# Turning the attention probabilities as two halves of 64 queries on the upper and lower rows of the array

## The chip, the cores and the metric

The kernel runs on one core of a Trainium2 chip. The metric is the device time of one execution, in microseconds. Times come from repeated runs; the profile is one further execution recorded by the hardware profiler.

## The reference

Pooled attention over 8 batches, 8 heads, 576 queries and head size 64, with keys and values averaged over groups of 8 (72 keys), then two layers of 4608 tokens, 512 wide, with a hidden width of 2048:

```python
k_p = k.reshape(B, H, Sp, pool, D).mean(axis=3)      # Sp = 72
v_p = v.reshape(B, H, Sp, pool, D).mean(axis=3)
scores = scale * np.matmul(q, k_p.transpose(0, 1, 3, 2))
attn = exp(scores - max); attn = attn / (sum(attn) + 1e-09)
x = (attn @ v_p) as 4608 x 512
h = x @ w_in;  g = h * (1.0 / (1.0 + np.exp(-h)));        x = g @ w_out
h = x @ w_in2; g = h * np.clip(h + 3.0, 0.0, 6.0) / 6.0;  out = g @ w_out2
```

## The kernel before, in words

The two layers are worked in four passes (two halves of the hidden width per layer) of nine steps each, `STEPS` = 36. A step takes one block of 512 tokens: first eight chunks (the product with `w_in`, by a fast scheme with seven block products instead of eight, in two fp32r parts each; lines 628 to 630), then 32 units (the product with `w_out`, three matmuls each; lines 714 to 716 in layer one, 720 to 722 in layer two).

The attention of batch s+1 is laid between the chunks and units of step s, for s = 0 to 6. A table written out by hand (`PLAN`, and `PLAN_FIRST` for step 0) says at which place of a step which event stands. A batch is five query tiles, `ROWS = [128, 128, 128, 128, 64]`: four full ones and a fifth of 64 queries. The events of a tile are "qt" (queries transposed, line 729), "s" (scores, line 736), "exp", "norm" (VectorE, lines 1332 to 1338), "pt" (`transpose_p`, line 745) and "pv" (`values`, line 753). The attention of batch 0 stands ahead of all steps, in `attend_first` (`first_turn` calls `transpose_p`), and the fifth tile of batch 0 is finished inside step 0.

`transpose_p` turns the probabilities `p_sb` of a tile, 8 heads of (queries x 72 keys), so that the keys lie on partitions. Each head is one fp32 transpose on TensorE: the probabilities are the weights (queries x 72 columns), the identity is the moving operand. Heads 0 to 3 go to one PSUM bank, heads 4 to 7 to a second one, and `pt_done` counts up when a bank is full:

```python
for g in range(2):
    for h in range(GH):
        last = nc.tensor.transpose(banks[g][:SP, h * P:h * P + rows], p_sb[:rows, tile % CT, GH * g + h, :],
                                   ident[:rows, :rows])
    last.then_inc(pt_done, 1)
```

ScalarE copies each bank to `pt` (line 1044; line 1094 for batch 0), and `values` then multiplies each head by the pooled values, even heads into the lower and odd heads into the upper 64 partitions of one bank, which are the two column halves of the array. ScalarE then copies that result to `x_raw` (line 1061) where the next step needs it, and to `x_out` (line 1066), which it sends to DRAM itself (line 1068).

In `PLAN` the first full tile is turned at place U+9 and its values follow at U+12; the other full tiles and the fifth are turned right behind the values of the tile before (U+12, U+15, U+18, U+21), and their own values follow three units later. In `PLAN_FIRST` the distance between "pt" and "pv" is two units from tile 0 on.

Of the kernel before, what the change touches and what calls it, by code (L numbers as in the profile page):

```python
# [10 lines left out]
B, H, S, D = 8, 8, 576, 64  # L11
POOL = 8
SP = S // POOL
DM = H * D
DF = 2048
P = 128
# [2 lines left out]
HB = BLK // 2  # L19
NB = B * S // BLK  # L20
GH = H // 2

# [8 lines left out]
CT = 5  # L33
# [140 lines left out]
def build(nc, q, k, v, w_in1, w_out1, w_in2, w_out2, out):  # L174
# [15 lines left out]
    with ctx:  # L190
        def sb(stack, name, shape, dt=fp32):
            return stack.enter_context(nc.sbuf_tensor(name, shape, dt))
# [26 lines left out]
        pt_first = sb(first_q, "pt_first", [SP, 2, H, P])  # L219
# [15 lines left out]
        ident = sb(att, "ident", [P, P])  # L235
# [5 lines left out]
        p_sb = sb(att, "p_sb", [P, CT, H, SP])  # L241
        pt = sb(att, "pt", [SP, H, P])
# [17 lines left out]
        banks = ab + zw + xy + acc  # L260
        first_q_bank = [ab[0], xy[0], xy[1], acc[0], acc[1]]
        first_s_banks = [(ab[0], ab[1]), (xy[0], zw[0]), (xy[1], zw[1]), (ab[0], ab[1]), (acc[0], acc[1])]
        first_p_banks = [(xy[0], zw[0]), (xy[1], zw[1]), (xy[0], zw[0]), (xy[1], zw[1])]
# [35 lines left out]
        pt_done = sem("pt_done")  # L299
# [69 lines left out]
        def first_value(h, heads=1):  # L369

            at = h % GH * D
            return w1_sum0[:SP, 2 + h // GH, 3, at:at + heads * D]

# [248 lines left out]
        def _(pe):  # L622
# [116 lines left out]
                        last.then_inc(s_done, 1)  # L739

            def transpose_p(tile, banks):
                rows = ROWS[tile % CT]
                for g in range(2):
                    for h in range(GH):
                        last = nc.tensor.transpose(banks[g][:SP, h * P:h * P + rows], p_sb[:rows, tile % CT, GH * g + h, :],
                                                   ident[:rows, :rows])
                    last.then_inc(pt_done, 1)

# [151 lines left out]
        def _(act):  # L900
# [117 lines left out]
            def attend(e):  # L1018
                kind, t = e[0], e[1]
                if kind == "kt":  # L1020
                    act.wait_ge(kt_done, t + 1)
                    if t == 1:
                        act.wait_ge(s_done, 2 * CT)
                    src = ab[0][:, :NK * SP].rearrange("p (j r) -> p j r", r=SP)
                    nc.scalar.copy(kt[:D, :, :SP], src[:D])
                    nc.scalar.copy(kt[D:, :, SP:], src[D:]).then_inc(bank_read[0], 1)
                elif kind == "qt":
                    rows = ROWS[t % CT]
                    n = t - CT
                    bank = banks_of(e)[0]  # L1030
                    act.wait_ge(qt_done, t + 1)
                    if t + 2 < TILES:
                        act.dma_start(q_raw[:ROWS[(t + 2) % CT], n % 2], q_rows(t + 2)).then_inc(q_loaded[n % 2], 16)
                    nc.scalar.copy(qt[:, :, :rows], banks[bank][:].rearrange("p (j r) -> p j r", r=P)[:, :, :rows])\
                        .then_inc(bank_read[bank], 1)
                elif kind == "exp":
                    exps(t, e[2])
                elif kind == "pt":
                    rows = ROWS[t % CT]
                    for g in range(2):  # L1040
                        bank = acc[g] if t == FIRST else banks[banks_of(e)[g]]
                        copied = first_pt_copied if t == FIRST else bank_read[banks_of(e)[g]]
                        act.wait_ge(pt_done, 2 * t + g + 1)
                        nc.scalar.copy(pt[:, GH * g:GH * (g + 1), :rows],
                                       bank[:SP].rearrange("r (h p) -> r h p", p=P)[:, :, :rows]).then_inc(copied, 1)
                elif kind == "pv":
                    b, c = t // CT, t % CT
                    rows = ROWS[c]
                    if t == FIRST:
                        bank, copied, count = acc[0], first_x_copied, CT  # L1050
                    else:
                        n = banks_of(e)[0]
                        bank, copied, count = banks[n], bank_read[n], BEFORE["pv", t, n] + 1
                    src = bank[:].rearrange("p (j r) -> p j r", r=P)
                    act.wait_ge(pv_done, t + 1)
                    if DIRECT[t]:
                        at, first, width = DIRECT[t]
                        act.wait_ge(x_split, 4 * max(b, 1))
                        if b <= 1:
                            act.wait_ge(x_first_stored, 64)  # L1060
                        nc.scalar.copy(x_raw[:, :, at:at + width], src[:, :, first:first + width]).then_inc(x_direct, 1)
                    if t > FIRST:
                        act.wait_ge(x_stored, 16 * (t - FIRST))
                    else:
                        act.wait_ge(x_first_stored, 64)
                    nc.scalar.copy(x_out[:, :, :rows], src[:, :, :rows]).then_inc(copied, 1)
                    act.wait_ge(copied, count)
                    act.dma_start(x_rows[:, :, b * S + c * P:b * S + c * P + rows], x_out[:, :, :rows])\
                        .then_inc(x_stored, 16)

            def attend_first():
                act.wait_ge(ident_ready, 2)
                act.wait_ge(zeroed, 1)
                nc.scalar.activation(ssum[:, 0, :1], ident[:, :1], ACT.Exp)

                def copy_q(c):
                    rows = ROWS[c]
                    act.wait_ge(qt_done, c + 1)
                    nc.scalar.copy(qt_fifth[:, :, :rows] if c == FIRST else qt_first[:, c],
                                   first_q_bank[c][:].rearrange("p (j r) -> p j r", r=P)[:, :, :rows])\  # L1080
                        .then_inc(first_qt_copied, 1)

                def exp(c):
                    rows = ROWS[c]
                    act.wait_ge(first_s_read, 2 * c + 2)
                    nc.scalar.activation(p_sb[:rows, c % CT], p_sb[:rows, c % CT], ACT.Exp, scale=float(D) ** -0.5 / POOL)\
                        .then_inc(exp_done, 1)

                def copy_p(c):
                    for g in range(2):  # L1090
                        act.wait_ge(pt_done, 2 * c + g + 1)
                        if c >= 2:
                            act.wait_ge(pv_done, c - 1)
                        nc.scalar.copy(pt_first[:, c % 2, GH * g:GH * (g + 1), :],
                                       first_p_banks[c][g][:SP].rearrange("r (h p) -> r h p", p=P))\
                            .then_inc(first_pt_copied, 1)

                def copy_x(c):
                    act.wait_ge(pv_done, c + 1)
                    src = first_v_bank[c][:].rearrange("p (j r) -> p j r", r=P)  # L1100
                    nc.scalar.copy(x_raw[:, :, c * P:(c + 1) * P], src).then_inc(first_x_copied, 1)
                    if c >= 2:
                        nc.scalar.copy(x_out[:, 2 * (c - 2):2 * (c - 1), :], src[:, 0:2]).then_inc(first_x_kept, 1)

                copy_q(0)
                act.wait_ge(kt_done, 1)
                src = acc[1][:, :NK * SP].rearrange("p (j r) -> p j r", r=SP)
                nc.scalar.copy(kt[:D, :, :SP], src[:D]).then_inc(first_kt_copied, 1)
                nc.scalar.copy(kt[D:, :, SP:], src[D:]).then_inc(first_kt_copied, 1)
                copy_q(1)  # L1110
                copy_q(2)
                exp(0)
                copy_q(3)
                exp(1)
                exp(2)
                copy_p(0)
                act.wait_ge(v_summed, 2)
                nc.scalar.copy(first_value(GH, GH), acc[1][:SP, 2 * P:]).then_inc(v_copied, 1)
                copy_p(1)
                round_w1(0, 0)  # L1120
                exp(3)
                copy_x(0)
                round_w1(0, 1)
                copy_p(2)
                copy_x(1)
                copy_p(3)
                round_x_first()
                copy_x(2)
                copy_q(FIRST)
                copy_x(3)  # L1130
                round_x_second()
                act.wait_ge(k_next_summed, 2)
                act.wait_ge(kt_done, 1)
                nc.scalar.copy(k_pool[:, GH:], ab[0][:SP, 2 * P:].rearrange("r (h d) -> r h d", d=D)).then_inc(k_next_copied, 1)
                round_x_last()
                round_w1(0, 2)

            attend_first()
            for s in range(STEPS):
                ps, blk = divmod(s, NB)  # L1140
                for place in range(END + 1):
# [7 lines left out]
                    else:  # L1149
# [4 lines left out]
                        if place in (2, 3, 6, 7):  # L1154
                            p = CHUNKS[place][1]
# [274 lines left out]
```

## Time and profile before

| | us |
|---|---|
| median of 3 runs (1703.26 to 1704.2) | 1703.68 |
| the profiled execution's own time | 1705.6 |
| its span, first to last instruction | 1703.8 |
| PE busy | 1686.2 (99%) |
| weight loads busy | 1519.0 (89%) |
| VectorE busy | 1040.7 (61%) |
| ScalarE busy | 726.5 (43%) |
| GpSimd busy | 351.9 (21%) |

An engine's busy time counts overlapping instructions once. A matmul's recorded duration is the time through the pipeline, so what a group of matmuls costs is read from the distance of starts in the timeline: from the start of the group to the start of what follows. In shapes such as "64*72 64x64" the weights are 64 partitions by 72 columns, and the moving operand is 64 partitions by 64 columns. An fp32 matmul that isn't a transpose is recorded twice, once for each pair of its passes, so the eight heads of `values` stand as x16.

### The profile page before, as it was taken

Reading aid. Unit: us, or ns where it says so; the run is one execution under the profiler, and the core shown is the slowest. Engines: PE = TensorE matmul, PEld = TensorE weight load, DVE = VectorE, ACT = ScalarE, POOL = GpSimd, SP = SyncE. Lnnn points to the kernel's source line nnn. Section 1 sums busy time; section 2 is a strip of 40 time slices with the busy share of each in tenths; the row PEclk is TensorE's granted clock in tenths of the full one; section 3 lists DMA queues with packets and bytes.
Section 4 is the critical chain, followed back from the end, with each engine's and each line's share of the span. In section 5 each row is a group of like instructions: output and inputs, shape, how many; then the busy total and the mean of one; then the engine's idle time right before and its main releaser. Section 6 shows DMA issues by size and latency. Waiting matters only on the chain.

```text
span 1703.8 us, 27465 instructions
## 1 busy us (share of the span) xinstructions
PE 1686.2 (99%) x11096; PEld 1519.0 (89%) x11096; DVE 1040.7 (61%) x1568; ACT 726.5 (43%) x1183; POOL 351.9 (21%) x443
## 2 busy tenths in 40 slices
PE   8999999999999999999999999999999999999999
PEld 7888988998899999999999899999998899999998
DVE  7757656656656555555557655555557666666664
ACT  4655555555544533333334434343335433333332
POOL 6655534634206300000006200000006200000000
PEclk7899999999999999999999999999999999999999
DMA  8243333443212322222223211111112322222221
GB/s 211 77 119 102 109 97 106 113 120 101 76 47 99 124 75 75 75 75 75 77 79 130 91 53 54 53 53 54 44 61 88 117 77 79 77 78 78 78 79 49
DMA packets 129838, 145.83 MB, mean 86 GB/s; under 512 B 47536, under 2 KB 74416, under 8 KB 129712
## 3 DMA queue, kind: packets, MB, share of 16 engines
q1 hardware_dynamic: 79968, 127.95, 22.9%
q10 hardware_dynamic: 49744, 16.13, 3.8%
q8 instruction: 88, 1.44, 0.4%
q14 instruction: 38, 0.31, 0.1%
HBM read 96.86 MB, written 47.19 MB: 85 GB/s over the span
## 4 chain that ended last, share of the span: by engine, by line
PE 95%; DVE 3%; ACT 1%; issue 1%; DMA 0%; POOL 0%; ACTq 0%; DVEq 0%; POOLq 0%
PE zw L628 8%; PE zw L629 8%; PE zw L630 8%; PE xy L628 6%; PE xy L630 6%; PE xy L629 6%; PE acc L714 6%; PE acc L716 5%; PE acc L715 5%; PE acc L720 4%; PE acc L721 4%; PE acc L722 4%; PE att L720 4%; PE att L722 4%; PE att L721 4%; PE att L716 2%
## 5 line engine op out<-in xcount | busy, mean ns | idle before, releaser
L1217 DVE TENSOR_TENSOR g_lo<-g_raw,g_hi 128x1024 fp32r<-128x1024 f32 x144 | 194.8, 1355 | 9.4 <-ACT g_raw L920 9.4
L908 ACT COPY x_sum<-xy 128x256 f32<-128x256 f32 x144 | 52.4, 365 | 293.8 <-PE xy L630 293.5
L1182 DVE TENSOR_TENSOR x_sum<-xy,x_sum 128x256 f32<-128x256 f32 x144 | 60.5, 420 | 189.6 <-ACT x_sum L908 189.6
L628 PE MATMUL xy<-xr_hi,w1r_hi 128*128 128x256 f32 x576 | 166.0, 288 | 0.6 <-DVE x_sum L1182 0.6
L533 POOL TENSOR_TENSOR w_sum<-w_raw 128x256 f32<-128x256 f32 x16 | 16.6, 1036 | 715.9 <-DMA w_raw<-in_moe_w_in_dram 715.9
L630 PE MATMUL xy<-xr_hi,w1r_lo 128*128 128x256 f32 x576 | 163.4, 284 | 0.0
L629 PE MATMUL xy<-xr_lo,w1r_hi 128*128 128x256 f32 x576 | 163.3, 283 | 0.0
L714 PE MATMUL acc<-g_hi,w_hi 128*128 128x512 f32 x400 | 162.2, 405 | 0.0
L1206 DVE TENSOR_TENSOR g_raw<-zw,x_sum 128x512 f32<-128x512 f32 x144 | 99.0, 688 | 95.6 <-PE zw L630 95.6
L716 PE MATMUL acc<-g_hi,w_lo 128*128 128x512 f32 x400 | 156.4, 391 | 0.0
L715 PE MATMUL acc<-g_lo,w_hi 128*128 128x512 f32 x400 | 156.2, 390 | 0.0
L547 POOL TENSOR_TENSOR kv_stage<-kv_stage 72x256 f32<-72x256 f32 x104 | 86.6, 833 | 159.7 <-DMA kv_stage<-in_v_dram 131.6
L1232 DVE SCALAR_TENSOR_TENSOR g_raw<-relu,g_raw 128x768 f32<-128x768 f32 x72 | 70.8, 983 | 72.9 <-ACT relu L937 72.9
L720 PE MATMUL acc<-w_hi,g_hi 128*128 128x512 f32 x288 | 113.0, 392 | 0.0
L628 PEld LDWEIGHTS xy<-xr_hi,w1r_hi 128*128 128x128 f32 x576 | 110.7, 192 | 2.4 <-DVE x_sum L1182 1.0
L721 PE MATMUL acc<-w_lo,g_hi 128*128 128x512 f32 x288 | 112.8, 392 | 0.0
L722 PE MATMUL acc<-w_hi,g_lo 128*128 128x512 f32 x288 | 112.5, 391 | 0.0
L720 PE MATMUL att<-w_hi,g_hi 128*128 128x512 f32 x288 | 112.0, 389 | 0.0
L721 PE MATMUL att<-w_lo,g_hi 128*128 128x512 f32 x288 | 112.0, 389 | 0.0
L722 PE MATMUL att<-w_hi,g_lo 128*128 128x512 f32 x288 | 112.0, 389 | 0.0
L629 PEld LDWEIGHTS xy<-xr_lo,w1r_hi 128*128 128x128 f32 x576 | 110.7, 192 | 1.4
L630 PEld LDWEIGHTS xy<-xr_hi,w1r_lo 128*128 128x128 f32 x576 | 110.7, 192 | 0.0
(209 smaller groups left out, 4882.1 us busy)
## 6 DMA issues: line engine op xcount, KB each, us to landing
partial<-y_stage SPq DMA_DIRECT2D x72, 256.0 KB, 2.1
y_part<-partial SPq DMA_DIRECT2D x18, 1024.0 KB, 5.9
x_raw<-first_layer_t SPq DMA_DIRECT2D x18, 1024.0 KB, 7.8
x_raw<-attended_t SPq DMA_DIRECT2D x10, 1024.0 KB, 8.2
first_layer_t<-y_stage SPq DMA_DIRECT2D x36, 256.0 KB, 2.0
out_dram<-y_stage SPq DMA_DIRECT2D x36, 256.0 KB, 2.0
w_raw<-in_moe_w_in_dram SPq DMA_DIRECT2D x16, 512.0 KB, 4.2
kv_stage<-in_v_dram SPq DMA_DIRECT2D x56, 144.0 KB
```

The costliest lines, as they stand in the source:

```text
L547: nc.gpsimd.tensor_tensor(src[:, :4 * D], src[:, :4 * D], src[:, 4 * D:], ALU.add).then_inc(kv_added, 1)
L628: nc.tensor.matmul(dst, s_hi[i], m_hi[i], start=first and i == 0, stop=False, skip_group_check=True)
L629: nc.tensor.matmul(dst, s_hi[i], m_lo[i], start=False, stop=False, skip_group_check=True)
L630: last = nc.tensor.matmul(dst, s_lo[i], m_hi[i], start=False, stop=i == 1, skip_group_check=True)
L714: nc.tensor.matmul(dst, w[0], g[0], start=f == 0, stop=False)
L715: nc.tensor.matmul(dst, w[0], g[1], start=False, stop=False)
L716: last = nc.tensor.matmul(dst, w[1], g[0], start=False, stop=f == NF - 1)
L720: nc.tensor.matmul(dst, g[0], w[0], start=f == 0, stop=False)
L721: nc.tensor.matmul(dst, g[0], w[1], start=False, stop=False)
L722: last = nc.tensor.matmul(dst, g[1], w[0], start=False, stop=f == NF - 1)
L1206: nc.vector.tensor_tensor(dst, src, u2[:, p % 2].unsqueeze(1).to_broadcast([P, 2, HB]), ALU.add)\
L1217: nc.vector.tensor_tensor(g_lo[:, p], g_raw[:, p % 2], g_hi[:, p].bitcast(fp32), ALU.subtract)\
```

## The change

A full tile is turned head by head as two transposes: queries 0 to 63 (partitions 0 to 63 of `p_sb`) into bank 0, queries 64 to 127 (partitions 64 to 127) into bank 1. Each bank then holds all eight heads, 64 columns a head. `pt_done` counts up twice at the end of the tile instead of once in the middle and once at the end. ScalarE's two copies of a tile read 72 x 512 contiguous columns as before and write eight runs of 64 with a step of 128. The fifth tile of 64 queries is turned as before, with its heads packed 64 columns apart in the bank.

```diff
+HP = P // 2
...
             def transpose_p(tile, banks):
                 rows = ROWS[tile % CT]
+                if rows == P:
+                    for h in range(H):
+                        for g in range(2):
+                            half = slice(g * HP, (g + 1) * HP)
+                            last = nc.tensor.transpose(banks[g][:SP, h * HP:(h + 1) * HP], p_sb[half, tile % CT, h, :],
+                                                       ident[half, half])
+                            if h == H - 1:
+                                last.then_inc(pt_done, 1)
+                    return
                 for g in range(2):
                     for h in range(GH):
-                        last = nc.tensor.transpose(banks[g][:SP, h * P:h * P + rows], p_sb[:rows, tile % CT, GH * g + h, :],
+                        last = nc.tensor.transpose(banks[g][:SP, h * HP:(h + 1) * HP], p_sb[:rows, tile % CT, GH * g + h, :],
                                                    ident[:rows, :rows])
                     last.then_inc(pt_done, 1)
...
                         act.wait_ge(pt_done, 2 * t + g + 1)
-                        nc.scalar.copy(pt[:, GH * g:GH * (g + 1), :rows],
-                                       bank[:SP].rearrange("r (h p) -> r h p", p=P)[:, :, :rows]).then_inc(copied, 1)
+                        src = bank[:SP].rearrange("r (h p) -> r h p", p=HP)
+                        if rows == P:
+                            nc.scalar.copy(pt[:, :, HP * g:HP * (g + 1)], src).then_inc(copied, 1)
+                        else:
+                            nc.scalar.copy(pt[:, GH * g:GH * (g + 1), :HP], src[:, :GH]).then_inc(copied, 1)
...
-                        nc.scalar.copy(pt_first[:, c % 2, GH * g:GH * (g + 1), :],
-                                       first_p_banks[c][g][:SP].rearrange("r (h p) -> r h p", p=P))\
+                        nc.scalar.copy(pt_first[:, c % 2, :, HP * g:HP * (g + 1)],
+                                       first_p_banks[c][g][:SP].rearrange("r (h p) -> r h p", p=HP))\
                             .then_inc(first_pt_copied, 1)
```

The turns keep their places on TensorE. Below is TensorE's order in step 1, around the values of the first tile and the turn of the second (`xy` and `zw` are PSUM banks, `v_pool` the pooled values), first of the kernel before:

```order
L716 MATMUL acc<-g_hi,w_lo 128x512
L753 MATMUL xy<-pt,v_pool 64x128 x8
L745 MATMUL zw<-ident,p_sb 72x128 x8
L714 MATMUL acc<-g_hi,w_hi 128x512
L715 MATMUL acc<-g_lo,w_hi 128x512
```

and of the changed kernel, whose lines stand one to twelve further down:

```order
L717 MATMUL acc<-g_hi,w_lo 128x512
L765 MATMUL xy<-pt,v_pool 64x128 x8
L750 MATMUL zw<-ident,p_sb 72x64 x16
L715 MATMUL acc<-g_hi,w_hi 128x512
L716 MATMUL acc<-g_lo,w_hi 128x512
```

Eight transposes of 128 columns have become sixteen of 64; both banks there are `zw` banks, written in turn. TensorE's order ahead of the steps, at the first tile of batch 0, where the two banks are `xy0` and `zw0`, was

```order
L821 MATMUL acc<-v_first,ident 72x128 x8
L745 MATMUL xy<-ident,p_sb 72x128 x4
L745 MATMUL zw<-ident,p_sb 72x128 x4
L821 MATMUL acc<-v_first,ident 72x128 x8
```

and begins in the changed kernel with

```order
L833 MATMUL acc<-v_first,ident 72x128 x8
L750 MATMUL xy<-ident,p_sb 72x64
L750 MATMUL zw<-ident,p_sb 72x64
```

the last two rows eight times over. The other engines keep their order and their waits.

## Rows read from the trace of the kernel before

**Rows 1.** The page: its first part and its chain of waits.
```profile
PE 1686.2 (99%) x11096; PEld 1519.0 (89%) x11096; DVE 1040.7 (61%) x1568; ACT 726.5 (43%) x1183; POOL 351.9 (21%) x443
...
PE 95%; DVE 3%; ACT 1%; issue 1%; DMA 0%; POOL 0%; ACTq 0%; DVEq 0%; POOLq 0%
```

**Rows 2.** Timeline of PE, step 1, second tile: start us, us, engine, line, shapes, count.
```profile
156.21 1.09 PE L753 MATMUL xy<-pt,v_pool 72*64 72x128 f32 x16
157.24 1.07 PE L745 MATMUL zw<-ident,p_sb 128*72 128x128 f32 x8
...
158.37 0.40 PE L715 MATMUL acc<-g_lo,w_hi 128*128 128x512 f32 x1
```

**Rows 3.** The same, step 1, first tile.
```profile
152.95 0.39 PE L716 MATMUL acc<-g_hi,w_lo 128*128 128x512 f32 x1
153.18 1.03 PE L745 MATMUL zw<-ident,p_sb 128*72 128x128 f32 x8
...
154.28 0.39 PE L715 MATMUL acc<-g_lo,w_hi 128*128 128x512 f32 x1
```

**Rows 4.** The same, step 1, fifth tile: its turn behind values.
```profile
168.54 1.09 PE L753 MATMUL xy<-pt,v_pool 72*64 72x128 f32 x16
169.56 0.64 PE L745 MATMUL zw<-ident,p_sb 64*72 64x64 f32 x8
170.13 0.50 PE L714 MATMUL acc<-g_hi,w_hi 128*128 128x512 f32 x1
170.47 0.40 PE L715 MATMUL acc<-g_lo,w_hi 128*128 128x512 f32 x1
```

**Rows 5.** The same, step 1, the fifth tile's values, in two column halves.
```profile
172.07 0.39 PE L716 MATMUL acc<-g_hi,w_lo 128*128 128x512 f32 x1
172.39 0.69 PE L753 MATMUL xy<-pt,v_pool 72*64 72x64 f32 x16
173.01 0.50 PE L714 MATMUL acc<-g_hi,w_hi 128*128 128x512 f32 x1
173.34 0.39 PE L715 MATMUL acc<-g_lo,w_hi 128*128 128x512 f32 x1
```

**Rows 6.** Timeline of PE ahead of the steps: sums of v, undivided array.
```profile
21.08 1.91 PE L821 MATMUL acc<-v_first,ident 72*72 72x128 f32 x16
```

**Rows 7.** Timelines of PE up to 69.8 us and up to 72 us: the same turn.
```profile
69.53 0.47 PE L745 MATMUL acc<-ident,p_sb 64*72 64x64 f32 x5
...
69.53 0.64 PE L745 MATMUL acc<-ident,p_sb 64*72 64x64 f32 x8
```

**Rows 8.** Weight loads by line: ns min/median/max, first and last start, forms.
```profile
L729 PEld LDWEIGHTS xy<-ident,q_raw x32: 134/137/140, 82.0 to 445.3; 64*128 64x128 f32 x28, 128*128 128x128 f32 x4
L745 PEld LDWEIGHTS acc<-ident,p_sb x8: 110/112/113, 69.5 to 69.9; 64*72 64x72 f32 x8
```

**Rows 9.** Timelines of ACT and PE, step 1, second tile, up to its values.
```profile
158.87 1.07 ACT L1044 COPY pt<-zw 72x512 f32<-72x512 f32 x2 [0.45 <-ACT x_out L1066]
...
160.32 0.55 PE L753 MATMUL xy<-pt,v_pool 72*64 72x128 f32 x6
```

**Rows 10.** The same, step 0, third tile.
```profile
102.13 1.07 PE L745 MATMUL zw<-ident,p_sb 128*72 128x128 f32 x8
...
103.76 1.06 ACT L1044 COPY pt<-zw 72x512 f32<-72x512 f32 x2 [0.45 <-ACT x_out L1066]
...
104.97 0.44 PE L753 MATMUL xy<-pt,v_pool 72*64 72x128 f32 x4 [0.37 <-ACT pt L1044]
```

**Rows 11.** Timeline ahead of the steps: PE and DVE, third and fourth tile.
```profile
28.58 1.07 PE L745 MATMUL xy<-ident,p_sb 128*72 128x128 f32 x4 [0.40 <-DVE p_sb L1338]
30.44 1.97 PE L753 MATMUL att<-pt_first,w_sum 72*64 72x128 f32 x16
30.65 1.12 DVE L1338 TENSOR_TENSOR p_sb<-p_sb,ssum 128x576 f32<-128x576 f32 x1
32.34 1.07 PE L745 MATMUL xy<-ident,p_sb 128*72 128x128 f32 x4
36.10 0.69 PE L729 MATMUL acc<-ident,q_fifth 64*128 64x64 f32 x4
36.71 1.97 PE L753 MATMUL att<-pt_first,w_sum 72*64 72x128 f32 x16
```

**Rows 12.** Windows: length, busy time by engine, granted clock, DMA share, GB/s.
```profile
24.40:51.60 27.20, 26.80 (x150) 22.86 (x151) 23.98 (x26) 16.88 (x28) 21.53 (x20) 0.50 0.53 149
65.40:68.60 3.20, 3.20 (x17) 3.20 (x17) 3.20 (x3) 2.65 (x5) 3.12 (x3) 0.50 0.63 158
```

**Rows 13.** Timeline of PE in step 0, where it waits longest.
```profile
64.58 0.66 PE L729 MATMUL att<-ident,q_raw 128*128 128x128 f32 x4 [3.12 <-DVE p_sb L1324]
```

## The prediction

> **What bounds the kernel now.** I read the page first. TensorE is busy 99% of the span, and the chain that ended last is TensorE for 95% of it [rows 1]. So an edit on TensorE counts nearly one for one wherever TensorE doesn't wait, and work on the other engines counts only where TensorE waits for it. The share of busy time says nothing of what a small matmul costs, so next I read TensorE's timeline around each kind of turn, from start to start. In step 1 the second tile's turn starts at 157.24 and the unit that follows has its second matmul at 158.37: 1.13 us for the turn and the first matmul [rows 2]. A first tile, which comes behind a unit and not behind values, takes 1.33 us from the unit's last matmul (152.95) to the next unit's second (154.28) [rows 3]. The fifth tile, 8 transposes of 64 columns on 64 rows, takes 169.56 to 170.47, 0.91 us [rows 4].
>
> There are 32 full tiles: 4 in batch 0, ahead of the steps, and 4 in each of steps 0 to 6.
>
> **What the change does, part by part.**
>
> *The turns of steps 0 to 6.* Eight transposes of 128 columns become sixteen of 64. The number of columns moved is the same, so if the instructions ran one after the other nothing would be won. What can win is that the upper and lower rows work at the same time. No row shows two row halves at work together; the nearest rows show two column halves. Undivided, 16 records of 128 columns take 1.91 us [rows 6]; `values`, 16 such records spread over two column halves, take 1.09 us [rows 2]. So halves of the array do run side by side in this kernel, at almost half the time. `values` of the fifth tile are 16 records of 64 columns in pairs, which is just the shape of the new turn: 0.62 us to the next unit's first matmul, 0.95 us to its second (172.39 to 173.34) [rows 5]. The other end is the fifth tile's turn, which is 8 such transposes in 0.91 us: with a perfect partner for each the new turn costs the same 0.91.
>
> A turn behind values (second to fourth tile) so goes from 1.13 to between 0.91 and 0.95 us: 0.18 to 0.22 saved, I take 0.20. That is little, because the divided array has to be left again: the first matmul behind the fifth tile's turn costs more than behind a full one. Behind the unit's last matmul, the first tile's turn goes from 1.33 us to 1.27 (172.07 to 173.34 is the same passage for `values` [rows 5]), or a little less: 0.06 to 0.10 saved, I take 0.08, since there the array is divided and joined again where before it never was.
>
> The Trainium skill (TensorEngine Tiling (Array Packing), Key Properties) speaks against the change: "Mode switching requires drain". The trace agrees: eight transposes at 0.057 us (below) and a unit's matmul at 0.23 make 0.69 us, and the fifth tile's turn takes 0.91, so passages cost 0.22. Without them 25 turns would save 5.5 us more than the sum below.
>
> *What hides and what doesn't.* `values` of a tile need both of ScalarE's copies. In step 1 the copies of the second tile begin at 158.87, behind the copies of the first tile's result and the sending of it, not behind the turn, and end at 159.94; `values` start at 160.32 [rows 9], 0.38 us later. In step 0 they start at 104.97, and there they wait: the copies end at 104.82, and the shortest distance is 0.15 [rows 10]. So from step 1 on a turn can become shorter by about 0.23 us before TensorE has to wait for ScalarE; the 0.20 just fits. In step 0 the second, third and fourth tile are bound by ScalarE already, and their saving is worth nothing: it comes back as a longer wait for `pt`.
>
> Both counts of `pt_done` now come at the end of the turn. Before, the first bank was full half way; the new turn as a whole ends about when that was, since it needs half the array time, so ScalarE starts no later. Copies have the same 512 columns on 72 partitions: nothing. 256 more instructions and weight loads are in the queue: nothing, since `values` of the fifth tile pass at the same rate.
>
> Sum: 6 steps x 3 tiles x 0.20 = 3.6; 7 first tiles x 0.08 = 0.6; step 0's other three 0. **4.2 us** saved, from 3.7 to 4.7 by the ends.
>
> *The turns of batch 0.* These run at half the clock (0.50 from 24.4 to 51.6) [rows 12]. The first two are followed by waits for VectorE's probabilities and give nothing. The third goes from 28.58 to the values at 30.44: 1.86 us [rows 11]. Four transposes of 64 columns and the passage to `values` take 0.61 there (36.10 to 36.71); with four more pairs at 0.11, twice the full-clock 0.057, the new turn is some 1.05 us. So 0.8 us each for the third and fourth. VectorE's last norm ends at 31.77, while TensorE would be ready at 31.5, so the two are worth 1.4 to 1.6 us of time at half the clock. All up to 51.6 runs at half the clock anyway, so this is 0.7 to 0.8 us of work at full clock. Behind it VectorE and ScalarE are almost fully busy with the first block, and TensorE ends by waiting 3.12 us for VectorE at 64.58 [rows 13]; if nothing passes through them the gain is 0. I take 0.8, ends 0 and 1.6.
>
> Just behind that wait the clock is halved once more for 3.2 us and a little [rows 12], which costs half of that, 1.7 us. If the wait moves, this fall may not come, or another may. That is 1.7 us either way, and not in the sum.
>
> **Sum:** 4.2 + 0.8 = 5.0 us. The profiled execution took 1705.6 us and would become 1700.6; the median of the runs is 1703.7, so 1698.7 us, 0.29% less. A measurement of this kernel tells about 0.2%, 3.4 us, from no change.
>
> **Rivals.**
>
> *The row halves take turns (slower).* If the lower half's transpose can't start while the upper one runs, sixteen transposes pass at the fifth tile's pace. Of one of those turns the first five end after 0.47 us and all eight after 0.64 [rows 7], 0.057 us each, so eight more add 0.45. A turn behind values costs 1.36 instead of 1.13, 0.23 more; a first tile's loses 0.35. 18 x 0.23 + 7 x 0.35 = 6.6, batch 0 about nothing, step 0's others hidden: 1710.3 us. It decides from the point at which a pair needs more than 0.082 us (where 0.20 is used up over eight pairs, 0.025 each). For it: no row shows row halves together, and these are fp32 transposes, not products. Against: the halves differ in partitions and in banks, while column halves, which share the partitions they read, do overlap. The Trainium skill (TensorE: Matmul & The Clock Gate, LDWEIGHTS) gives 72/1.2 = 60 ns for each load of 72 columns; if the loads of a pair followed each other that would be an estimate of 120 ns a pair and this rival's outcome. The rows don't bear the figure out as it stands: the fifth tile passes at 57 ns with 72 columns each, a shade less.
>
> *The weight loads of a pair follow each other, but quicker (no change).* A load of 128 columns on 64 rows is recorded with 137 ns, one of 72 with 112 [rows 8]: 0.45 ns a column, so two loads of 72 are some 65 ns, against the 57 to 60 a pair on which my saving rests, and perhaps 70 with what lies between. Eight times 6 to 11 ns take 0.05 to 0.09 off each turn: 18 x 0.13 + 0 + 0.6 gives about 3 us, 1700.8. For it: every transpose brings its own load, and nothing else in the kernel loads so densely on row halves. Against: loads for different partitions.
>
> *ScalarE becomes the bound.* If the copies start later than I think (their output is in runs of 64), the spare 0.23 us is gone and 18 turns give nothing: 0.6 + 0.8 saved, 1702.3. Against: they start behind the result's copies, over half a us after the turn's end.
>
> **How the numbers follow.** My forecast 0.66 (0.60 of it over 0.2%, as the half-clock stretch can take 1.7 away); it may also reach 1696 if the second fall of the clock goes. Loads or ScalarE limit: 0.17, within 0.2% mostly. Row halves take turns: 0.17, slower. Faster 0.64, same 0.19, slower 0.17. The range goes from 1696.0 (4.7 + 1.3 + 1.7 saved) to 1703.0 (ScalarE's case, less some batch 0 saving) and leaves out the slower case.
>
> **What would show it.** In the profile after: a turn of 16 with 64*72 weights starting right behind values, and the next unit's second matmul 0.91 to 0.95 us behind its start; 1.36 would be the slower rival, 1.0 the loads. Starts of a pair a few ns apart. In steps 1 to 6 the distance from one tile's values to the next falls from 4.11 to about 3.9, with no wait for `pt`; in step 0 the waits for `pt` grow by 0.2 us each. Ahead of the steps the fourth turn starts near 31.6 instead of 32.34. A pair pitch over 0.082 us, or waits for `pt` in steps 1 to 6, would make me wrong.

## The result and the profile after

| | before | after |
|---|---|---|
| median, us | 1704.10 (10 runs, 1702.2 to 1705.61) | 1698.05 (10 runs, 1697.51 to 1700.08) |
| ratio | | 0.9967, 95% interval 0.9958 to 0.9975 |
| span of the profiled execution | 1703.8 | 1696.0 |
| PE busy, instructions | 1686.2, 11096 | 1674.4, 11352 |

The changed kernel is 6 us faster (4.3 to 7.2 by the interval). The forecast was 5.0 us.

First the timeline of TensorE in the profile of the changed kernel, step 1: the first tile's turn behind a unit, and the second tile's turn behind values (start us, us, engine, line, tiles, shapes, count).

```profile
149.86 0.39 PE L717 MATMUL acc<-g_hi,w_lo 128*128 128x512 f32 x1
150.18 0.64 PE L750 MATMUL zw<-ident,p_sb 64*72 64x64 f32 x16
150.75 0.50 PE L715 MATMUL acc<-g_hi,w_hi 128*128 128x512 f32 x1
151.08 0.40 PE L716 MATMUL acc<-g_lo,w_hi 128*128 128x512 f32 x1
...
153.03 1.09 PE L765 MATMUL xy<-pt,v_pool 72*64 72x128 f32 x16
154.06 0.64 PE L750 MATMUL zw<-ident,p_sb 64*72 64x64 f32 x16
154.63 0.50 PE L715 MATMUL acc<-g_hi,w_hi 128*128 128x512 f32 x1
154.97 0.40 PE L716 MATMUL acc<-g_lo,w_hi 128*128 128x512 f32 x1
...
156.92 1.09 PE L765 MATMUL xy<-pt,v_pool 72*64 72x128 f32 x16
```

Sixteen transposes last 0.64 us, exactly what eight lasted in [rows 4]: each upper one has a lower one beside it that costs nothing. In the single records a pair starts 3 to 5 ns apart and pairs follow at 0.056 us. From the turn's start to the second matmul behind it are 0.91 us (154.06 to 154.97), against 1.13 in [rows 2]. The first tile's passage is 1.22 us (149.86 to 151.08), against 1.33 in [rows 3]. Three times 0.22 and once 0.11 are 0.77 us a step.

The distance from one tile's values to the next has gone from 4.11 us [rows 2, 9] to 3.89 (153.03 to 156.92). What ScalarE does in that time, from its timeline in the same profile:

```profile
154.17 0.58 ACT L1076 COPY x_raw<-xy 128x512 f32<-128x512 f32 x1 [2.26 <-PE xy L765]
154.66 0.59 ACT L1081 COPY x_out<-xy 128x512 f32<-128x512 f32 x1
155.28 0.37 ACTq L1083 DMA_DIRECT2D attended_t<-x_out  x1
155.69 1.06 ACT L1058 COPY pt<-zw 72x512 f32<-72x512 f32 x2 [0.44 <-ACT x_out L1081]
```

The copies of the turned probabilities take 1.06 us for the two, as before, although they now write runs of 64. They end at 156.75, and the values start at 156.92, 0.17 us later. The shortest distance seen is 0.15 [rows 10]. So there is no wait, and 0.02 us more would have made one.

In step 0 the savings did come back as waits. From the list of waits of TensorE (us in total, times, longest), before:

```profile
PE xy L745 <- DVE p_sb L1338: 2.2, 3, 1.4
...
PE xy L753 <- ACT pt L1044: 1.0, 3, 0.4
```

and after:

```profile
PE xy L750 <- DVE p_sb L1353: 3.9, 3, 2.5
...
PE att L730 <- DVE p_sb L1339: 3.2, 1, 3.2
...
PE xy L765 <- ACT pt L1058: 1.6, 3, 0.6
```

The three waits for `pt` have gone from 1.0 us in sum to 1.6. The long wait for VectorE in step 0 has stayed (3.1 us before). The waits of batch 0's turns for VectorE, 2.2 us before and 3.9 after, differ as much between two executions of one kernel: 3.5 and 3.7 in two more profiles of the kernel before, 1.4 in a second one of the changed kernel.

In batch 0 the clock is halved, and there the third turn and the start of its values are, in the profile after,

```profile
27.87 0.32 PE L750 MATMUL xy<-ident,p_sb 64*72 64x64 f32 x1 [2.54 <-DVE p_sb L1353]
...
28.87 1.97 PE L765 MATMUL att<-pt_first,w_sum 72*64 72x128 f32 x16
```

1.00 us apart, against 1.86 in [rows 11].

Where the 7.8 us between the two profiles lie shows in where the steps begin. Here are the starts of step 1 from the timelines of PE, the line of the last unit of step 0 and the first chunk: of the kernel before,

```profile
118.77 0.39 PE L716 MATMUL acc<-g_hi,w_lo 128*128 128x512 f32 x1
119.00 0.28 PE L628 MATMUL xy<-xr_hi,w1r_hi 128*128 128x256 f32 x1
```

and of the changed one:

```profile
115.68 0.39 PE L717 MATMUL acc<-g_hi,w_lo 128*128 128x512 f32 x1
115.91 0.28 PE L629 MATMUL xy<-xr_hi,w1r_hi 128*128 128x256 f32 x1
```

Read the same way, step 7 begins at 476.48 before and at 468.71 after. So 3.1 us are won ahead of step 1 and 4.7 in steps 1 to 6 (0.78 a step); from there to the end the two differ by less than 0.1 us. Whether the 3.1 us belong to the change is a question for the experiments.

### The profile page after: what moved, and what is told of

Its sections match the earlier page's. It is cut to its first block, busy times and chain, and to the rows that moved or that the text cites. A ratio compares the mean times of both kernels' runs of the same rounds, so it can differ in the third digit from the quotient of the medians.

```text
span 1696.0 us, 27977 instructions
## 1 busy us (share of the span) xinstructions
PE 1674.4 (99%) x11352; PEld 1504.7 (89%) x11352; DVE 1043.5 (62%) x1568; ACT 726.3 (43%) x1183; POOL 354.2 (21%) x443
## 4 chain that ended last, share of the span: by engine, by line
PE 93%; DVE 4%; ACT 1%; issue 1%; DMA 0%; POOL 0%; ACTq 0%; SPq 0%; DVEq 0%; POOLq 0%
PE zw L629 8%; PE zw L631 8%; PE zw L630 8%; PE acc L715 6%; PE xy L629 6%; PE xy L631 6%; PE xy L630 6%; PE acc L716 5%; PE acc L717 5%; PE acc L721 4%; PE acc L722 4%; PE acc L723 4%; PE att L722 4%; PE att L723 4%; PE att L721 4%; PE att L716 2%
```

## The experiments

### Only the steps, only batch 0

The first two kernels leave one part of the turns whole. `split(tile)` says which tiles are divided, and the others are turned and copied with the old lines:

```diff
+def split(tile):
+    return tile % CT == CT - 1 or (tile >= CT)
...
+                if not split(tile):
+                    for g in range(2):
+                        for h in range(GH):
+                            last = nc.tensor.transpose(banks[g][:SP, h * P:(h + 1) * P], p_sb[:, tile % CT, GH * g + h, :],
+                                                       ident[:])
+                        last.then_inc(pt_done, 1)
+                    return
...
```

The second kernel has `(tile < CT)` in place of `(tile >= CT)`. Steps only:

> Only the turns of steps 0 to 6 are divided; batch 0, ahead of the steps, is turned whole as before. Theory (the steps carry the gain, 0.78 us in each of steps 1 to 6 as the distance of step starts in the trace of after shows, 59.58 to 58.80): 4.7 us less than before, ratio 0.9972, about 1699.4 us. Rival (batch 0 carries half of it, by shifting the half-clock stretches; the trace of after reaches step 1 3.1 us sooner): only some 3 us less, ratio 0.9982, about 1701.

Measured: 1700.23 us median against 1704.08, ratio 0.9979, interval 0.9970 to 0.9988. Steps 1 to 6 take 352.96 us in its profile, against 357.48 before and 352.80 after: all but 0.2 us of the steps' gain is there. The interval holds the theory's 0.9972 and the rival's 0.9982 alike.

Batch 0 only:

> Only batch 0's four tiles are turned in halves, steps 0 to 6 as before. Theory: 0.8 to 1.3 us less than before, ratio 0.9992 to 0.9995. Rival (clock): about 3 us less, ratio 0.9982. In the profile the fourth turn starts about 0.8 to 1.2 us sooner than before, at 31.1 to 31.6.

Measured: 1703.13 us median, ratio 0.9994, interval 0.9985 to 1.0003 (one execution of 5824 us, unlike all others, doesn't move the median). Steps 1 to 6 take 357.52 us, and the fourth turn begins at 31.59, within the 31.1 to 31.6 expected. So batch 0 is worth about 1 us, not 3, and by itself can't be told from nothing. The rival's 3 us are outside the interval, though not by much: it reaches to 2.6.

### How much of the 3.1 us is one execution's luck

Two more profiles of the kernel before, each with the same question.

> The kernel before, unchanged, once more in profile, to see how much of the 3.1 us by which the trace of after reached step 1 sooner (115.9 against 119.0) is the change and how much is where the half-clock stretches fell in one execution. Theory (the change is worth 0.8 to 1 us there, the rest is the clock): step 1 begins between 116.5 and 118.5 in at least one of two looks. Rival (the change is worth all of it): 119.0 in both.

> As the run before it: a second look at the same kernel, with the same two expectations.

| profile | step 1 begins, us | clock falls, us | clock rises, us | steps 1 to 6, us |
|---|---|---|---|---|
| before | 119.00 | 24.3 | 51.6 | 357.48 |
| before, second | 116.46 | 28.0, 38.2 | 31.4, 48.5 | 357.50 |
| before, third | 117.64 | 29.3 | 49.8 | 357.49 |
| after | 115.91 | 27.5 | 48.0 | 352.80 |
| after, second | 118.38 | 20.9 | 51.6 | 352.80 |

The start of step 1 scatters over 2.5 us in either kernel, while steps 1 to 6 repeat within 0.02 us here (352.89, 352.96 and 353.10 in the profiles of three experiments that have the same turns there). The stretches at half clock lie differently in each execution. How much of the scatter is theirs is not shown. The mean is 117.7 before and 117.1 after. The two profiles whose stretches are most alike, before (third) and after, both 20.5 us long, begin step 1 1.7 us apart. The other experiments' profiles add 117.5 with batch 0 whole, and 116.3, 116.0, 115.8 and 120.7 with it divided, the last with a wait of 2.3 us at a fifth tile. So a good part of the 3.1 us was luck, and how much isn't settled: what the change is worth there lies near 1 us. The profile that I forecast from had the latest start of the five. This is why the difference of the profiles (7.8 us) is larger than that of the medians (6.0). The second profile after is one of the kernel run again:

> The changed kernel itself once more, on the chip on which the next three run, so that differences of 1 to 3 us are read on one chip: 1698.0, ratio 0.9965.

Measured: 1699.15 us median, ratio 0.9971, interval 0.9960 to 0.9982.

### Step 0's turns

> As after, but the four full tiles turned inside step 0 are turned whole, with the old layout. Theory (three of them end in a wait for ScalarE's copy and only the first saves 0.1 us): no more than 0.3 us slower than after. Rival (their savings count as in the other steps): 0.7 us slower. In the profile the waits of the values for pt are back at 1.0 us in sum, from 1.6 in after.

The edit is `return tile % CT == CT - 1 or (tile < CT or tile >= 2 * CT)` in `split`. Measured: 1699.26 us median, against 1699.15 for the changed kernel on the same chip; ratio 0.9975, interval 0.9966 to 0.9985. The waits for `pt` behind whole turns are back at 1.0 us:

```profile
PE xy L776 <- ACT pt L1074: 2.3, 1, 2.3
...
PE xy L776 <- ACT pt L1069: 1.0, 3, 0.4
```

The lower row is the one that is meant. The 2.3 us in the upper one are a wait at the fifth tile that no other profile has; this profiled execution was the slowest of its ten. The difference of 0.1 us is what the theory says, but the rival's 0.7 us lie within what these intervals can't tell apart. What speaks for the theory is the waits: what three of step 0's turns save, TensorE waits again.

### The same transposes in another order

```diff
-                    for h in range(H):
-                        for g in range(2):
+                    for g in range(2):
+                        for h in range(H):
```

> As after, but all eight upper-row transposes of a tile first, then all eight lower-row ones: same instructions, same banks, only the order within the turn differs. Theory (two transposes run together only when they stand next to each other on different row halves): each turn takes 0.45 us more than in after, 1.36 us to the next unit's second matmul instead of 0.91; 25 turns, 11 us, so 1709 to 1711 us, ratio 1.003 to 1.004 to before. Rival (TensorE takes the other half's transposes from its queue ahead of time): as after, 0.9967.

Measured: 1705.26 us median, ratio 1.0005, interval 0.9996 to 1.0014. So the same instructions in another order give up the whole gain, but lose only 7 us against the changed kernel, not 11. Timeline of TensorE of this kernel, step 1, second tile:

```profile
155.23 0.90 PE L750 MATMUL zw<-ident,p_sb 64*72 64x64 f32 x16
156.06 0.50 PE L715 MATMUL acc<-g_hi,w_hi 128*128 128x512 f32 x1
156.40 0.40 PE L716 MATMUL acc<-g_lo,w_hi 128*128 128x512 f32 x1
```

The turn costs 1.17 us (155.23 to 156.40): more than the whole one's 1.13 and less than the 1.36 expected of sixteen one after the other. That is 0.26 more than in the changed kernel, for 25 turns 6.5 us, about what was lost. The starts of the single records tell why. Their distances in ns are 86, 55, 56, 56, 7, 49, 39, 17, 39, 17, 39, 56, 55, 56, 56: the first four upper transposes go alone, the next four have one of the lower half beside each, and the last four lower ones go alone. Twelve places instead of sixteen. So the first lower transpose, the ninth in the program, starts beside the fifth upper one, ahead of three that stand before it. TensorE does look ahead, but only about four transposes far. Both my theory (no overlap) and the rival (full overlap) were wrong; the truth lies between.

### The scores in row halves

If pairs come free for the turn, they might for the scores, where half of `kt` is zeros so that one product of 128 rows serves two heads.

```diff
                 for j in range(NK):
-                    last = nc.tensor.matmul(banks[j // 2][:rows, j % 2 * 2 * SP:(j % 2 + 1) * 2 * SP],
-                                            src[:, j, :rows], kt[:, j, :], start=True, stop=True)
-                    if j % 2:
-                        last.then_inc(s_done, 1)
+                    for g in range(2):
+                        half = slice(g * D, (g + 1) * D)
+                        last = nc.tensor.matmul(banks[g][:rows, j * SP:(j + 1) * SP], src[half, j, :rows],
+                                                kt[half, j, g * SP:(g + 1) * SP], start=True, stop=True)
+                        if j == NK - 1:
+                            last.then_inc(s_done, 1)
...
+                    to = p_sb[:rows, tile % CT].rearrange("p (j two) r -> p two j r", two=2)[:, g]
-                    nc.vector.tensor_tensor(p_sb[:rows, tile % CT, GH * g:GH * (g + 1), :], src,
+                    nc.vector.tensor_tensor(to, src,
```

> As after, and the scores too in row halves: per pair of heads two products of 64 rows by 72 columns into two banks instead of one product of 128 rows by 144 columns with half of kt zero. Each record now loads 128 weight columns on a row half. Theory (row halves run together, weight loads included): 8 pairs of records at 0.062 us for 8 records at 0.122, 0.49 less and 0.2 more for the passages, 0.28 less per tile; 34 tiles in steps 0 to 6 give 8 to 10 us, 1688 to 1690 us, ratio 0.991 to 0.992. Rival (loads of a pair follow each other): a pair needs 0.12 us, no gain and the passages on top, 1704 us or so.

Measured: 1700.78 us median, ratio 0.9978, interval 0.9968 to 0.9987. That is 2.7 us more than the changed kernel's 1698.05 and 1.6 more than the 1699.15 of its second measurement, and the intervals overlap. In the profiles steps 1 to 6 take 353.83 us against 352.80. So the steps cost 1 us more, and the gain expected isn't there. Timeline of TensorE, step 1, one tile's scores in halves:

```profile
137.75 0.28 PE L631 MATMUL zw<-xr_hi,w1s_lo 128*128 128x256 f32 x1
137.96 1.11 PE L739 MATMUL att<-kt,qt 64*128 64x72 f32 x16
139.00 0.66 PE L730 MATMUL acc<-ident,q_raw 128*128 128x128 f32 x4
139.42 0.36 PE L629 MATMUL xy<-xr_hi,w1r_hi 128*128 128x256 f32 x1
```

and the same place in the profile of the changed kernel:

```profile
137.28 0.28 PE L631 MATMUL zw<-xr_hi,w1s_lo 128*128 128x256 f32 x1
137.40 1.15 PE L737 MATMUL att<-kt,qt 128*128 128x144 f32 x8
138.38 0.60 PE L730 MATMUL acc<-ident,q_raw 128*128 128x128 f32 x4
138.74 0.36 PE L629 MATMUL xy<-xr_hi,w1r_hi 128*128 128x256 f32 x1
```

The halves take as long as the whole (1.11 against 1.15), and the passages come on top: from the chunk's last matmul to the first of the next 1.67 us, against 1.46. Three tiles of a step lose these 0.21 us each; the fourth, whose scores stand between units, gains 0.09 and the fifth 0.48 in the same two profiles, so that a step loses less than 0.1 us, and waits in three of the steps make up the rest of the 1 us. Pairs follow at 0.112 us, not at 0.062. In the fifth tile, with 64 queries and so 64 weight columns, pairs did follow at 0.063. So something grows with the weight columns, but the rival's reason (loads of a pair one after the other) is only one of two possible.

### Pairs by themselves

Behind the warm-up stand series of small matmuls on the identity, in two banks that nobody uses then (the two helpers `turn` and `mult` are left out here, and the comments are added):

```diff
...
+                for n in (72, 96, 112, 128):
+                    for i in range(8):
+                        for g in range(2):
+                            turn(g, n, i)          # transpose: n weight columns, 64 moved, row half g, bank g
+                for n in (72, 128):
+                    for i in range(8):
+                        turn(0, n, i)
+                for n in (72, 96, 112, 128):
+                    for i in range(4):
+                        for g in range(2):
+                            mult(g, n, 72, i)      # fp32 product: n weight columns, 72 moved
+                for i in range(4):
+                    mult(0, 128, 72, i)
+                for g in range(2):
+                    for i in range(16):
+                        turn(g, 72, i)
+                for i in range(6):
+                    nc.tensor.transpose(zw[0][:72, :P], ident[:, :72], ident[:])
+                    for g in range(2):
+                        turn(g, 72, i)
+                for i in range(6):
+                    nc.tensor.transpose(zw[0][:72, :P], ident[:, :72], ident[:])
```

> As after, with series of small matmuls on the identity behind the warm-up, ahead of everything else; their results are overwritten. Pairs on row halves: transposes with 72, 96, 112, 128 weight columns and 64 moving ones, one half alone with 72 and 128, fp32 products with 72, 96, 112, 128 weight columns and 72 moving ones, one half alone with 128; then 16 transposes on each half one after the other, whole transposes with a pair between each two, and whole ones alone. Theory A (weight loads of the two halves share one path, some 0.44 ns a column): pairs of transposes 0.056, 0.084, 0.098, 0.112 us, products the same with 72 columns at 0.063 to 0.070. Theory B (loads of the halves are parallel, and what made the scores slow is that both halves write all 128 partitions of PSUM, or the fp32 products): transposes stay at 0.056 to 0.062 for all widths, and only products rise, or a step comes between two widths. The passage between whole and divided costs 0.2 us there and back, so a whole transpose and a pair take some 0.36 us together.

Lines by form of the products in the stretch from 13.2 to 16.8 us (busy us, mean ns of one):

```profile
L873 PE MATMUL zw<-ident 64*128 64x72 f32 x24 | 2.0, 272 | 0.0
L873 PE MATMUL zw<-ident 64*112 64x72 f32 x16 | 1.0, 258 | 0.0
L873 PE MATMUL zw<-ident 64*96 64x72 f32 x16 | 0.9, 245 | 0.0
L873 PE MATMUL zw<-ident 64*72 64x72 f32 x16 | 0.8, 229 | 0.0
```

and of the transposes from 10.2 to 12.1 us, which don't differ so:

```profile
L869 PE MATMUL zw<-ident 64*72 64x64 f32 x16 | 0.6, 220 | 0.0
L869 PE MATMUL zw<-ident 64*112 64x64 f32 x16 | 0.6, 216 | 0.0
L869 PE MATMUL zw<-ident 64*96 64x64 f32 x16 | 0.6, 216 | 0.0
```

From the starts of the single records, in ns from one pair (or one alone) to the next:

| weight columns | transposes, pair | one half alone | product records, pair | one half alone |
|---|---|---|---|---|
| 72 | 56 | 56 | 65 | |
| 96 | 56 | | 85 | |
| 112 | 56 | | 99 | |
| 128 | 62 | 62 | 112 | 112 |

Wherever both were measured, a pair costs what one half costs alone. So the two row halves load their weights side by side too, and theory A falls. What grows is the distance of the fp32 product's records, some 0.87 ns a weight column, on one half as on both; a transpose with 128 weight columns passes in 62 ns. The recorded weight loads grow alike: their medians for the four widths are 142, 162, 175 and 188 ns for products, 112, 123, 130 and 138 for transposes. So I put it down to the load of the product, which no run separates from the product itself. By that reading the undivided scores hide the load under 144 moved columns (0.122 us a record), and with 72 moved it stands bare. Of theory B the part on the products holds; 128 partitions of PSUM written by both halves are no hindrance, since one half alone is as slow.

The Trainium skill (TensorE: Matmul & The Clock Gate, LDWEIGHTS) gives columns/1.2 ns, which is 60, 80, 93 and 107 ns for the four widths. The products here agree within 6 ns, the transposes don't (62 for 128).

The sixteen transposes on each half one after the other again had four places in common and twelve alone at either end, 28 places for 32 transposes: the look-ahead doesn't depend on the length of the series. For the passages, the timeline where whole transposes and pairs take turns:

```profile
19.00 0.30 PE L894 MATMUL zw<-ident 128*72 128x128 f32 x1
19.23 0.25 PE L869 MATMUL zw<-ident 64*72 64x64 f32 x2
19.41 0.30 PE L894 MATMUL zw<-ident 128*72 128x128 f32 x1
19.65 0.25 PE L869 MATMUL zw<-ident 64*72 64x64 f32 x2
...
21.07 0.85 PE L898 MATMUL zw<-ident 128*72 128x128 f32 x6
```

One round takes 0.41 us. A whole transpose in its own series takes 0.109 and a pair 0.056, so the two passages cost 0.25 us, 0.12 each way. I had expected 0.2. Between units, at the first tile's turn, they cost more: 1.22 us less eight pairs at 0.056 and two unit matmuls at 0.23 leaves 0.31.

### A version that beats both

With 64 weight columns (0.87 times 64 is 56 ns, an estimate) the load should just hide under 72 moved columns, whose pairs followed at 0.063 us above. So the fifth tile's scores are worth dividing, and there the array is divided anyway: the queries fill half its columns (128*64 in the timeline below).

```diff
             def scores(src, tile, banks):
                 rows = ROWS[tile % CT]
+                if rows < P:
+                    for j in range(NK):
+                        for g in range(2):
+                            half = slice(g * D, (g + 1) * D)
+                            last = nc.tensor.matmul(banks[g][:rows, j * SP:(j + 1) * SP], src[half, j, :rows],
+                                                    kt[half, j, g * SP:(g + 1) * SP], start=True, stop=True)
+                            if j == NK - 1:
+                                last.then_inc(s_done, 1)
+                    return
...
```

VectorE's subtraction of the fifth tile writes the heads back in their old order, as in the run with all scores in halves.

> As after, and the scores of the fifth tiles alone (64 queries, so 64 weight columns) as products of 64 rows by 72 columns in row halves, which took 0.063 us a pair in the run with all scores in halves, against 0.122 a record undivided, with no more passages than before. Theory: 0.4 us less per fifth tile, 7 tiles, 3 us less than after: 1695 us, ratio 0.9948. Rival (the fifth tile's scores are followed by work that waits for VectorE): as after.

Measured: 1695.1 us median, ratio 0.9950 to before, interval 0.9937 to 0.9962; the changed kernel on the same chip 1699.15, and the slowest of these five runs (1696.21) is faster than its fastest of six (1697.82). Steps 1 to 6 take 350.47 us in its profile against 352.80, 0.39 a step. Timeline of TensorE at the fifth tile's scores, step 1, of this kernel

```profile
146.29 0.40 PE L717 MATMUL acc<-g_hi,w_lo 128*128 128x512 f32 x1
146.62 0.72 PE L740 MATMUL att<-kt,qt 64*64 64x72 f32 x16
147.27 0.50 PE L715 MATMUL acc<-g_hi,w_hi 128*128 128x512 f32 x1
147.60 0.39 PE L716 MATMUL acc<-g_lo,w_hi 128*128 128x512 f32 x1
```

and in the changed kernel at the same tile, a step later:

```profile
205.26 0.40 PE L717 MATMUL acc<-g_hi,w_lo 128*128 128x512 f32 x1
205.59 1.20 PE L737 MATMUL att<-kt,qt 128*64 128x144 f32 x8
206.71 0.50 PE L715 MATMUL acc<-g_hi,w_hi 128*128 128x512 f32 x1
```

0.65 us instead of 1.12 to the next unit, with 0.33 ahead of it in both. So a tile gains 0.47 us and a step only 0.39. The rival has that part: the first tile's turn now comes so early that it waits for VectorE's probabilities. From the timelines of VectorE and TensorE, step 1:

```profile
148.49 1.23 DVE L1365 TENSOR_TENSOR p_sb<-p_sb,ssum 128x576 f32<-128x576 f32 x1
149.22 0.40 PE L717 MATMUL acc<-g_hi,w_lo 128*128 128x512 f32 x1
149.86 0.64 PE L759 MATMUL zw<-ident,p_sb 64*72 64x64 f32 x16 [0.24 <-DVE p_sb L1365]
```

The turn starts 0.15 us behind the end of the norm and 0.64 behind the unit's last matmul, where it was 0.32 in the changed kernel. In four of the six steps it starts 0.15 behind the norm (in the changed kernel the shortest distance is 0.21). So VectorE's norm is what binds next at that place. The 4.0 us between the two medians are more than the 2.3 of steps 1 to 6 and another 0.4 for step 0; where the rest comes from is open.

Not tried: both halves of a head into one and the same bank, which would have kept the old layout. Whether two row halves can write one bank at once stays open here.

## Why the prediction was right, point by point

- **The turn behind values.** Forecast 0.91 to 0.95 us, taken as a saving of 0.20. Measured 0.91, 0.22 saved: the lower end, since a partner costs nothing. `values` of the fifth tile in [rows 5], from which the 0.95 came, are fp32 products, whose pairs pass a little slower than transposes.
- **The first tile.** Forecast 0.08, measured 0.11. Steps 1 to 6 so gave 4.7 us, where the forecast's terms for them make 4.1. The 0.6 us are the two sizes together: 18 turns by 0.02 more and 6 by 0.03 more.
- **The passages.** Read as 0.22 us from the fifth tile; alone they are 0.25, and 0.31 around a first tile's turn. They leave 0.22 of the 0.42 us that eight pairs save over eight whole transposes (8 times 0.109 less 8 times 0.056), and 0.11 at a first tile. The Trainium skill (TensorEngine Tiling (Array Packing), Key Properties) has it that a change of tiling mode drains TensorE. The traces agree in that each change costs time; what happens during it they don't show. That 25 turns would save 5.5 us more without the passages was wrong by the forecast's own next paragraph: from step 1 on a turn behind values could become shorter by 0.23 us only, of which 0.22 are used.
- **What hides.** The spare 0.23 us before ScalarE binds: measured use 0.22, 0.17 us left between copy and values where 0.15 is the least. Step 0's three turns behind values gave next to nothing, and their waits grew by 0.6 us in sum, as written. Not weighed was VectorE's norm ahead of the first tile's turn, which ended 0.21 us ahead of it at the least in the profile after, where 0.15 is the least seen anywhere; it bound in the version with the fifth scores divided.
- **Batch 0.** Forecast 0.8 us. The run with batch 0 alone says 1.0, the interval from 2.6 less to 0.5 more. The third and the fourth turn take 1.00 us each to their values (27.87 to 28.87 and 31.11 to 32.11, at half the clock), where 1.05 was forecast and 1.86 was measured before; so the turns themselves are as forecast. The fourth began at 31.11 instead of 32.34, sooner than the 31.6 written down, but the clock in that execution fell later too. What of it reaches the end is consistent with 0.8 and not shown. In the range, its low end took 1.3 us for batch 0 where the end given was 1.6.
- **The second fall of the clock** did not go away: it came in every profile listed, between 61 and 66 us, from 0.3 us before the end of the same wait to 0.9 behind it.
- **Rivals.** "The row halves take turns" is false as the change is written; the point at which a pair would cost more than 0.082 us was not reached (0.056). The order of the loops is what it depends on: with the halves one after the other the gain is gone. "Loads of a pair follow each other" is false: pairs of 72 and of 128 columns pass at the pace of one half alone. My 0.45 ns a column, read from the recorded durations of loads, was near what one half needs for a transpose (62 ns for 128 columns), but says nothing of two halves. "ScalarE becomes the bound" is false by 0.02 us.

The sum was 5.0 us, the medians say 6.0 with an interval of 4.3 to 7.2. Of the missing 1 us, 0.6 is in steps 1 to 6. The other 0.4 isn't placed: it is less than the scatter ahead of step 1 (2.5 us) and from step 7 to the end (1226.3 to 1227.3 in the five profiles). The mechanism was right, and that the measured gain lies within 1 us of the forecast owes nothing to two errors that cancel: each term measured in the steps is a little larger than forecast.

## What to carry to other kernels

Small fp32 transposes on at most 64 rows each can run in pairs on the upper and lower rows at the price of one, if the two stand next to each other in the program (all of these wrote two different banks; one bank was not tried). Count 0.25 to 0.31 us for dividing and rejoining the array, and find out first which copy or wait binds next, since that caps the gain. Before dividing products the same way, compare the columns moved with the weight columns: here records of fp32 products with 72 moved columns passed at 0.87 ns a weight column or more, so pairs won next to nothing at 128 weight columns (0.112 us a pair against 0.122 a whole record) and half the time at 64 (0.063). And when the effect is a few us, look at a stretch that repeats (six steps agreed within 0.3 us between executions) and not at the span, whose first 120 us scattered by 2.5.

## What the runs showed that I had not expected

- TensorE takes transposes for a free row half out of order, but only about four ahead: four places in common between two series of eight, and four between two of sixteen.
- With 128 weight columns on 64 rows, fp32 products of 72 moved columns pass at 112 ns and fp32 transposes of 64 at 62, and both at the same pace on one row half as on two at once.
- The next bound stood just behind the change at two places: ScalarE's copies 0.02 us from making a wait, and VectorE's norm 0.06 (0.21 us ahead of the turn, where 0.15 is the least).
- The unchanged kernel reached step 1 at 116.5, 117.6 and 119.0 us in three executions, with the stretch at half clock lying differently in each.
